# Attention, routing and two expert stages on one core: a pair's preparation moved from steps 2 to 4 to steps 1 to 3, and five filler products more

## What is computed

```python
scores = q @ k.T / 8                          # per head, 576 x 576
keep = scores >= max(scores) - tau            # per row
attn = exp(scores - max) * keep; attn /= sum(attn) + 1e-9
x = attn @ v                                  # 2304 x 512
x = moe(x)        # each token to the expert with the largest logit, two matmuls and a gate
out = (relu(h) + alpha * min(h, 0)) @ w_out   # h = x @ w_in
```

## Time and profile before

| | us |
|---|---|
| median of 3 runs | 1011.72 |
| lowest and highest | 1011.56, 1011.73 |
| the profiled execution, its own time | 1013.92 |
| its span in the trace | 1012.2 |
| TensorE busy | 1001.4 (99%) |
| VectorE busy | 529.3 (52%) |
| ScalarE busy | 388.9 (38%) |
| attention: pair 0's first scores | at 10.6 |
| pair 15's last scores end | at about 322 |

### The profile page before, as it was taken

One profiled execution on the slowest core, in us unless ns is written; L12 is line 12 of the kernel. 1 busy time (PEld: TensorE's weight loads), 2 busy tenths in 40 slices (PEclk: granted clock), 3 DMA queues, 4 the chain that ended last, 5 costly groups with the idle time before them and its releaser, 6 DMA issues.

```text
span 1012.2 us, 19467 instructions
## 1 busy us (share of the span) xinstructions
PE 1001.4 (99%) x6541; PEld 886.6 (88%) x6542; DVE 529.3 (52%) x1206; ACT 388.9 (38%) x814; POOL 337.6 (33%) x446
## 2 busy tenths in 40 slices
PE   9999999999999999999999999999999999999997
PEld 8999999999998788888888889999899999998996
DVE  5888888888988422222222237544444434444442
ACT  5777777777776232222232223211121211111111
POOL 2233344222131789999854542010010100100101
PEclk9999999999999999999999999999999999999999
DMA  5876777776671655566563435001001000000000
GB/s 124 222 166 168 189 192 176 189 191 164 157 190 42 219 196 195 206 213 205 181 198 129 130 126 160 1 32 32 1 32 32 32 15 17 31 0 0 32 1 31
DMA packets 103744, 116.69 MB, mean 115 GB/s; under 512 B 70380, under 2 KB 70412, under 8 KB 103156
## 3 DMA queue, kind: packets, MB, share of 16 engines
q1 hardware_dynamic: 88404, 87.52, 31.6%
q10 hardware_dynamic: 11120, 13.97, 4.4%
q0 software_dynamic: 4144, 14.20, 4.0%
HBM read 68.53 MB, written 19.12 MB: 87 GB/s over the span
## 4 chain that ended last, share of the span: by engine, by line
PE 95%; POOL 2%; DVE 1%; issue 1%; DMA 0%; ACT 0%; POOLq 0%; SPq 0%; DVEq 0%
PE bank L790 82%; PE bank L793 13%; POOL ring L690 1%; DVE neg_max L1563 0%; POOL ring L688 0%; DMA qraw<-in_q 0%; DVE probs L1571 0%; POOLq L89 0%; POOL out L783 0%; POOL x_sorted L731 0%; DVE X L1602 0%; ACT probs L1302 0%; ACT o_row L1527 0%; DVE emb_row L1757 0%; DVE X L1652 0%
## 5 line engine op out<-in xcount | busy, mean ns | idle before, releaser
L790 PE MATMUL bank<-x_hi,ring 128*128 128x384 f32 x768 | 210.7, 337 | 0.0
L790 PE MATMUL bank<-ring,g_hi 128*128 128x512 f32 x576 | 179.2, 392 | 0.0
L1504 ACT ACTIVATE g_hi<-act 128x384 fp32r<-128x384 f32 x96 | 50.4, 525 | 299.2 <-DVE act L1947 296.7
L690 POOL TENSOR_TENSOR ring<-stage,ring 128x2048 fp32r<-128x2048 f32 x32 | 147.2, 4600 | 4.8 <-POOL ring L688 0.2
L790 PEld LDWEIGHTS bank<-x_hi,ring 128*128 128x128 f32 x768 | 140.3, 188 | 3.5
L1944 DVE TENSOR_SCALAR neg<-bank,alpha_col 128x384 f32<-128x384 f32 x96 | 59.2, 617 | 150.9 <-PE bank L790 150.9
L790 PE MATMUL bank<-x_lo,ring 128*128 128x384 f32 x384 | 129.0, 336 | 0.0
L1302 ACT ACTIVATE probs<-bank,neg_max 128x576 f32<-128x576 f32 x144 | 102.8, 741 | 59.4 <-DVE neg_max L1563 59.4
L790 PEld LDWEIGHTS bank<-ring,g_hi 128*128 128x128 f32 x576 | 106.9, 188 | 18.6 <-DVE g_lo L1895 0.3
L1571 DVE SCALAR_TENSOR_TENSOR probs<-bank,thresh,probs 128x576 f32<-128x576 f32 x144 | 112.7, 816 | 14.2 <-ACT probs L1302 13.6
L1563 DVE TENSOR_REDUCE neg_max<-bank 128x1 f32<-128x576 f32 x144 | 104.1, 754 | 25.1 <-PE bank L790 24.2
(11 more groups left out here) (204 smaller groups left out, 1412.7 us busy)
## 6 DMA issues: line engine op xcount, KB each, us to landing
stage<-in_moe_w SPq DMA_DIRECT2D x26, 1024.0 KB, 5.3
k_st<-k_both SPq DMA_DIRECT2D x60, 288.0 KB, 5.2
x_row<-x_sorted ACTq DMA_DIRECT2D x23, 296.0 KB, 3.3
stage<-in_moe_w SPq DMA_DIRECT2D x12, 512.0 KB, 6.2
y_sorted<-y_row ACTq DMA_DIRECT2D x21, 256.5 KB, 2.9
q_st<-q_hi SPq DMA_DIRECT2D x30, 160.0 KB, 2.8
q_st<-q_lo SPq DMA_DIRECT2D x30, 160.0 KB, 2.9
qraw<-in_q SPq DMA_DIRECT2D x16, 256.0 KB, 3.3
```

Of the source, the lines that this page charges most:

```text
L690: nc.gpsimd.tensor_tensor(lo, src, hi.bitcast(F32), ALU.subtract).then_inc(piece_lo, 2)
L790: return nc.tensor.matmul(dst, lhsT, rhs, start=start, stop=stop)
L1504: nc.scalar.activation(g_hi[f % 3][:, :], act2[f % 2][:, :], ACT.Copy).then_inc(g_hi_ready, 1)
```

## The change

`group_of` gives, for every pair n but 0, steps 1, 2, 3 instead of 2, 3, 4 for the three groups of pair n + 2; pair 0 keeps steps 2, 3, 4. Since all three engines and the SP queue's waits hang on it, ScalarE's and VectorE's splits come in steps 2, 3, 4 of the same pair, and step 0 has none (but step 0 of pair 1, which takes group 2 turned in pair 0). The normalisation in step 0 goes ahead of the masks as in all other steps. One filler product is added behind the first small product, two between the turns of q and k of pair 1, and two behind these.

```diff
--- before.py
+++ after.py
@@ -395,8 +395,8 @@
 
             if (n, j) == (0, 0):
                 return 1, 2
-            m, g = n + 2, j - 2
-            return (m, g) if g >= 0 and m < PAIRS else None
+            m, g = n + 2, j - (1 if n else 2)
+            return (m, g) if 0 <= g < GROUPS_PREP and m < PAIRS else None
 
         def for_slots(eng, body, between=None):
 
@@ -806,6 +806,7 @@
             busy(FILL - 2)
             pe.wait_ge(taus_in, 32)
             mm(bank[:, M_BANK, 0:2], ones[0:1, :], taus[0:1, 0:2], True, True).then_inc(setup_pe, 1)
+            busy(1)
 
             def prep(n, par, half, g, b=QK_BANK):
 
@@ -1072,8 +1073,10 @@
             busy(FILL - 3, S_BANK[1] + 1)
             opening_scores()
             for g, b in enumerate(SECOND_BANKS):
+                if g:
+                    busy(2)
                 prep(1, 1, 0, g, b)
-            busy(FILL // 2)
+            busy(FILL // 2 + 2)
             for n in range(PAIRS):
                 pair(n, n % 2, n // 2)
             last_pair = PAIRS - 1
@@ -1697,8 +1700,7 @@
                     for g in range(3):
                         if (n, j) == route_unit(g, STEP_AT[g][7]):
                             route_step(g, 7)
-                    late = j == 0 and 0 < n < PAIRS - 1
-                    if not (static(n) and j < 4) and not late:
+                    if not (static(n) and j < 4):
                         normalise(*((n, j - 4) if j >= 4 else (n - 1, j + UNITS - 4)))
                     if (n, j) == (PAIRS - 1, 0):
                         dve.wait_ge(open_hi, 1)
@@ -1708,8 +1710,6 @@
                         scale_rows()
                     for h in heads_of(n, j):
                         mask(n, j, h)
-                    if late:
-                        normalise(n - 1, UNITS - 4)
                     if (n, j) == (0, 2):
                         place_params()
                     if not (static(n) and j == 0):
```

## The result

| | us |
|---|---|
| changed kernel, median of 5 | 1016.32 (1015.83 to 1018.32) |
| kernel before, median of 5 | 1011.72 (1011.56 to 1011.73) |
| ratio, with its 95% interval | 1.005 (1.0036 to 1.0063) |
| profiled execution after: own time, span | 1017.06, 1015.4 |

The change costs 4.6 us, outside the range of 1008.3 to 1013.2 and on the other side of the forecast.

What follows compares the result with a forecast made beforehand. TensorE, holding 95% of the chain that ended last, was taken to bound the kernel. Boundaries -1.6, new wait +0.8 and fillers +0.2 gave -0.6 on the median of 1011.72: 1011.1 us, range 1008.3 to 1013.2.

Steps and rivals of the forecast that it cites:

- The steady part: Boundaries into pairs 2 to 14: less waiting by TensorE, together -1.6 us (bounds -4.7 and +0.5).
- step 4's saving: Step 4 loses two transposes, 0.22 of TensorE work, but waiting for the second mask in step 0 takes it back.
- the rival of the delayed mask: Normalisation delays step 0's first mask, on which TensorE waits: 3.8 us slower, 1014.9; chance 0.08.
- that of step 4 for nothing: Nothing of step 4's 0.22 is lost, VectorE's round having more room: 2.9 us more gain, 1008.2; chance 0.18.
- the three boundaries with a routing step: Boundaries where VectorE has a routing step, with 0.1 more wait ahead of the scores: -0.24 us each.
- the two with a ranking product: Boundaries where ranking products push TensorE back and it had no wait: +0.22 us each.
- the second rival: Nothing of step 4's 0.22 is lost at 13 boundaries: 2.9 us more gain, 1008.2; chance 0.18.
- The one new wait: Pair 1: ScalarE waits for k's last transfer, landing at 49.9; costs TensorE 0.8 us once (bounds 0 and 1.6).
- signs of being wrong: Pair of 19.1 or less or above 19.45; no `k_st` wait in pair 1, or later ones; pair 0's products before 10.
- Into pair 14 the wait goes (-0.36) and nothing follows: Boundary into pair 14: TensorE's wait of 0.36 us disappears, with no cost set against it.
- The fillers: Start: first new filler costs +0.2 us on everything behind; the four others count 0 (bounds -0.9 and 0).
- the clock comes up sooner: Start: added filler closes the gap before 6.51, the clock rises earlier, 1.2 us gained, 1009.9; chance 0.25.

Runs made afterwards that it cites:

- experiment 3: Kernel before with only the normalisation of step 0 moved ahead of the masks: 1009.86, ratio 0.998 (0.997 to 0.999).
- experiment 2: Changed kernel without its five fillers, so moved turns and normalisation only: 1016.11, ratio 1.0043 (1.0026 to 1.0059) to the kernel before.
- experiment 7: Changed kernel with one piece of expert weights issued behind pair 2's spread on the SP queue: 1015.33, ratio 1.0013 to the kernel before.
- experiment 6: Kernel before with the new places of the turns in pairs 4 to 12 and nothing else: 1014.22, ratio 1.0002 (0.9991 to 1.0012).
- experiment 1: Kernel before with the five fillers alone: 1011.86, ratio 1.0001 (0.9991 to 1.0011).
- experiment 10: Changed kernel with expert weights behind pair 2's spread and pair 13's turns back in steps 2 to 4: 1014.71, ratio 1.0006 to the kernel before.
- experiment 8: Kernel before with the five fillers and the normalisation ahead of the masks, turns at old places: 1011.95, ratio 0.998 (0.997 to 0.999).

## Why the prediction was wrong

**The steady part held in its mechanism and in part in its sizes.** An ordinary boundary was to give 0.14, and those into pairs 4, 8 and 12 gave 0.13 to 0.15. Those into pairs 7 and 11 took 0.05 more instead, and the one into pair 3 0.19 more, with a cause that stays open. Its signs came as named: the scores of step 1 follow the transposes by 0.36 and take 1.13, those of step 0 take 1.37 (forecast 0.35, 1.16 and 1.38), so step 4's saving is lost as said, and VectorE's first mask of step 0 starts 1.64 behind the maxima. Neither the rival of the delayed mask nor that of step 4 for nothing came. Sizes were off where routing interferes as well: the three boundaries with a routing step gave 0.02 more, 0.26 less and 0 where 0.24 less each was said; the two with a ranking product gave nothing where 0.22 more was said. The sum is -1.0 for -1.6. (Two figures beside the sum were added wrongly: with the 0.22 counted at 12 boundaries, the lower bound is -4.3 and not -4.7, and the second rival 1008.5 and not 1008.2.) But the mechanism was read as one: the prediction gave the gain to both parts together, while the normalisation's place alone gives it all (1.9 us at the median, experiment 3).

**The step that failed is "The one new wait".** It put the cost at one wait of 0.8 us, for k's landing, and the wait for q's landing, at which pair 1 lost most, at nothing. The changed kernel's trace has 3.50 us of waiting for `q_st` on ScalarE, 2.71 of idle time on TensorE and 4.58 in all, and only 0.34 of waiting for `k_st`. Three splits move one step forward, and the prediction followed the landing only for k, because 49.9 was the last landing in the rows. q is split one step before k; ScalarE was free for it at 41.4, and the landing was at 44.85. The prediction should have asked the same of each group: when is it issued, when has it landed, when does ScalarE now come. The trace of before had what that takes but for the landing: the spread starts at 39.35, the last issue for `q_st` is the fourth, 1.86 later, at 41.21, and ScalarE would come at 43.6, behind the exponentials of step 2. With k's 6.0 from issue to landing as the upper bound that is a wait of 3.6 us, with the 2.9 of experiment 7 half a microsecond. The term belonged in the range at least. Of the signs of being wrong that were named two came: pair 0's products start before 10, and a pair takes above 19.45 (19.63 into pair 3). The prediction also used the TensorE times of the late start (k's turn at 50.2), in which this wait does not arise, as experiment 2 shows: there ScalarE waits for k until 49.51 (forecast 49.9), and for q not at all. At the median the start is the early one, TensorE comes 2 us sooner to an SP queue that comes only 0.3 to 1 us sooner.

**The clock was counted as a gain only.** The fall at 17 us was weighed for the fillers, but not as what may follow a new wait on the path. It makes most of 1.87 of the 4.58 us.

**Pair 14 was costed at nothing.** "Into pair 14 the wait goes (-0.36) and nothing follows" left out that ScalarE waits there for the last scatter, which may land late: 1.5 us in the changed kernel's trace on the first chip, nothing in that on the third. Pair 15's spread does move a step forward beside that scatter, but whether this is the cause stays open, as experiment 6 has the wait without it.

**The fillers** at +0.2 and 0 were right in substance; experiment 1 measures 0.1 with an interval of 1 us on either side. That the late start of the profiled execution was typical was wrong: it accounts for about the 2.2 us by which that execution stood above the median. So the rival "the clock comes up sooner" saw the trace rightly and had nothing to gain at the median. It took the clock's fall behind a gap of 0.88 as the cause; the Trainium skill ("TensorE: Matmul & The Clock Gate", "HAM oscillation — how this bites in real kernels") has the clock fall behind long waits. The runs do not settle this: in the three late starts the gap in the weight loads is 0.88 to 0.89 and the clock falls, in the two early ones without fillers it is 0.50 and 0.66 and the clock does not fall, so the gap and the late start came together each time.

## What to carry to other kernels

When a producer is moved one step earlier, list every buffer that its consumer overwrites and set the landing of the last reader's transfer against the new time, group by group, at the first and the last iteration too; the steady state hides it, since only where the move begins is the transfer still issued by the old schedule. Take a change with two parts apart before it is kept: here a reordering of one small VectorE operation gives 0.2% by itself, and the moved turns add nothing to it and cost on top. Compare a profiled execution with the median before its early microseconds are used.

## What the runs showed of the hardware

- A copy of 160 KB within the on-chip memory took 2.9, 4.4, 4.6 and 4.95 us from its issue to its landing in four executions, at the same place of the program, with the DMA engines 0.87 to 1.04 busy from 40 to 44 us. The last k transfer of the same spread took at most 5.5 us in experiment 1 and 7.1 in experiment 3, both with the turns at their old places. The spread of the changed kernel's times (1014.92 to 1019.11 on the third chip) goes with the clock: 1014.92 at a mean granted clock of 0.999, those above 1017.1 at 0.997.
- TensorE's clock fell to the lower level after 2.2, 2.5 and 2.7 us without work in pair 1 and stayed there for some 3 us, and did not after 1.68 (experiment 10) or 0.85 (experiment 7), each behind 20 us and more at the higher level; nor after 1.48 in pair 14 of the changed kernel.
- The last scatter of rows took 7.7 us to land in the changed kernel, with a spread begun 5.8 us ahead of it, and 7.0 in experiment 6 with one begun 2.7 ahead; it took 6.2 or less in experiment 8 with one begun 2.9 ahead, and 5.0 or less in the kernel before with one begun 1.7 ahead. So the spread's start alone does not decide it.
